# Linear attention by chunks and two gated layers: products regrouped by bank, and another bound in the test of the inputs

## The reference

```python
for t in range(S):
    state = alpha[:, :, t, :, None] * state + np.einsum('bhd,bhe->bhde', k[:, :, t], v[:, :, t])
    y[:, :, t] = np.einsum('bhd,bhde->bhe', q[:, :, t], state)
...
h = x @ w_in
g = P(h) / (Q(h) + 1e-06)
x = g @ w_out
h = x @ w_in2
solu = h * softmax(h)
out = layernorm(solu, g_ln) @ w_out2
```

## Time and profile before

| what | us |
|---|---|
| median of three runs | 815.07 |
| the profiled execution | 815.7 |
| its span, first to last instruction | 814.0 |
| busy in the span: PE | 785.0 (96%) |
| busy in the span: DVE | 689.2 (85%) |
| busy in the span: ACT | 607.9 (75%) |
| busy in the span: POOL | 313.2 (38%) |

### The profile page before, as it was taken

One profiled execution on the slowest core, in us unless ns is written; L12 is line 12 of the kernel. 1 busy time (PEld: TensorE's weight loads), 2 busy tenths in 40 slices (PEclk: granted clock), 3 DMA queues, 4 the chain that ended last, 5 costly groups with the idle time before them and its releaser, 6 DMA issues.

```text
span 814.0 us, 16268 instructions
## 1 busy us (share of the span) xinstructions
PE 785.0 (96%) x5378; PEld 728.5 (89%) x5378; DVE 689.2 (85%) x1248; ACT 607.9 (75%) x1258; POOL 313.2 (38%) x376
## 2 busy tenths in 40 slices
PE   5989999989889999999999999999999999999998
PEld 4777777779779999999999999999999999999988
DVE  4879999879999888988898888988898888988854
ACT  5778888678878776887678767876778677867743
POOL 4998886522223322332233322332333232323221
PEclk9999999999999999999999999999999999999999
DMA  8899999410000010001000100010001000000000
GB/s 182 204 231 230 236 229 206 126 46 0 30 2 1 11 41 1 10 11 39 0 10 10 39 10 0 10 39 10 0 10 39 10 0 10 11 10 1 11 20 30
DMA packets 113174, 42.96 MB, mean 53 GB/s; under 512 B 101616, under 2 KB 110960, under 8 KB 113136
## 3 DMA queue, kind: packets, MB, share of 16 engines
q1 hardware_dynamic: 110336, 33.04, 17.1%
q0 software_dynamic: 2800, 9.45, 3.9%
HBM read 33.04 MB, written 9.44 MB: 52 GB/s over the span
## 4 chain that ended last, share of the span: by engine, by line
PE 70%; DVE 13%; ACT 7%; issue 3%; SPq 3%; DMA 2%; POOL 0%; PEld 0%; ACTq 0%; DVEq 0%; PEldq 0%; POOLq 0%
PE h_ps L1024 18%; PE acc_ps L1050 17%; PE y_ps L1006 12%; PE z_ps L1068 12%; SPq L210 2%; PE chunks_y L299 2%; DVE work L1268 2%; PE chunks_y L307 2%; PE z_ps L1078 2%; DVE chunks_bp L453 2%; DVE rec L1260 2%; DVE den L1256 2%; ACT rec L1157 1%; ACT g_hi L1147 1%; DVE den L1273 1%
## 5 line engine op out<-in xcount | busy, mean ns | idle before, releaser
L1207 POOL TENSOR_TENSOR g_lo<-work,g_hi 128x384 fp32r<-128x384 f32 x128 | 130.8, 1022 | 401.5 <-ACT g_hi L1147 401.5
L1024 PE MATMUL h_ps<-x,w 128*128 (+1 forms) x1143 | 224.8, 340 | 5.8 <-DVE work L1278 4.3
L1050 PE MATMUL acc_ps<-g_hi,w 128*128 128x384 f32 x768 | 218.4, 338 | 2.2 <-POOL g_lo L1207 2.2
L1024 PEld LDWEIGHTS h_ps<-x,w 128*128 128x128 f32 x1143 | 200.4, 188 | 12.2 <-DVE work L1278 8.3
L1050 PEld LDWEIGHTS acc_ps<-g_hi,w 128*128 128x128 f32 x768 | 141.2, 188 | 2.8 <-POOL g_lo L1207 2.8
L1119 ACT ACTIVATE h<-h_ps 128x384 f32<-128x384 f32 x128 | 61.7, 482 | 99.0 <-PE h_ps L1024 98.8
L1050 PE MATMUL acc_ps<-g_lo,w 128*128 128x384 f32 x384 | 129.6, 338 | 0.0
L1273 DVE SCALAR_TENSOR_TENSOR den<-h,ncoef,den 128x384 f32<-128x384 f32 x128 | 78.6, 614 | 39.9 <-ACT den L1122 38.8
L1068 PE MATMUL z_ps<-w,x 128*128 128x512 f32 x396 | 99.9, 397 | 2.4 <-DVE lnT L1290 2.4
L1006 PE MATMUL y_ps<-w,lnT 128*128 128x384 f32 x528 | 99.9, 338 | 0.0
L1147 ACT ACTIVATE g_hi<-work 128x384 fp32r<-128x384 f32 x128 | 68.1, 532 | 38.2 <-DVE work L1268 35.0
(11 more groups left out here) (135 smaller groups left out, 1168.7 us busy)
## 6 DMA issues: line engine op xcount, KB each, us to landing
work<-in_alpha_dram SPq DMA_DIRECT2D x32, 144.0 KB, 3.7
chunks_xin<-in_q_dram SPq DMA_DIRECT2D x32, 144.0 KB, 3.4
chunks_xin<-in_k_dram SPq DMA_DIRECT2D x32, 144.0 KB, 4.1
chunks_vin<-in_v_dram SPq DMA_DIRECT2D x16, 288.0 KB, 4.0
wstage<-in_moe_w_in_dram POOLq DMA_DIRECT2D x9, 512.0 KB, 5.5
attention_out<-solu SPq DMA_DIRECT2D x32, 144.0 KB, 3.5
out_dram<-ysb SPq DMA_DIRECT2D x24, 192.0 KB, 1.8
x<-attention_out SPq DMA_DIRECT2D x7, 576.0 KB, 3.9
```

Of the source, the lines that this page charges most:

```text
L1024: mm = nc.tensor.matmul(h_ps[:, s % 2, 0:TT], w1[:, wz, kc, s * P:(s + 1) * P], xs[:, xz, kc, :], start=(n == 0), stop=(n == 3 * KC - 1))
L1050: mm = nc.tensor.matmul(acc_ps[:, dc, 0:TT], w2[:, wz, f, dc * P:(dc + 1) * P], rhs, start=(f == 0 and n == 0), stop=(f == FC1 - 1 and n = ...
L1207: nc.gpsimd.tensor_tensor(g_lo[:, 1 - o, :], gate[:, 1 - o, :], g_hi[:, 1 - o, :].bitcast(F32), ALU.subtract).then_inc(glo_done, 1)
```

## The change

- `y`'s second bank (chunks 3 to 5) holds the pair's heads in swapped places: head 0 in rows 64 to 111, head 1 in rows 0 to 47 (`y_row`). The rows in between that nothing writes any more are cleared once by DVE.
- On TensorE all of `within` comes first, then all of `before`, in the order of chunks 1, 4, 2, 5, 3, so that four products in a row use four different quarters of the array; `y_done` is raised once a pair.
- ACT copies `ktok` in one instruction of 672 columns and y in one of 768, instead of two each.
- The stores are four per pair, of 48 rows by 384, instead of two of 48 by 2 by 384.
- The test: exp(-80 * alpha) goes. In its place the sum of 1/b, taken by `accum_out` on the exp that computes 1/b anyway, is compared with 2^60. exp(60 * alpha) stays, and its bound becomes exp(60 * 1.05) where it was exp(60 * 1.35).
- POOL clears `seen` once at the start, and ACT and DVE wait for that; semaphore values follow the new counts; `ext` has another home.

```diff
-DECAY_MIN, DECAY_MAX = 0.71, 1.35
-LOW_STEEP, HIGH_STEEP = -80.0, 60.0
-LOW_MAX = math.exp(LOW_STEEP * DECAY_MIN)
-HIGH_MAX = math.exp(HIGH_STEEP * DECAY_MAX)
+DECAY_MAX = 1.05
+STEEP = 60.0
+HIGH_MAX = math.exp(STEEP * DECAY_MAX)
+RECIPROCALS_MAX = 2.0 ** 60
...
+        def y_row(j, z):
+
+            return (j ^ z) * HB
...
-            for j in range(2):
-                nc.sync.dma_start(
-                    scratch[bass.ds(m // PPB * 2, 2), bass.ds(m % PPB * (2 * D) + j * D, D), :].rearrange("o d t -> d o t"),
-                    halves(yout[j * HB:j * HB + D, :]),
-                ).then_inc(att_stored, 16)
+            for z in range(2):
+                for j in range(2):
+                    nc.sync.dma_start(
+                        scratch[bass.ds(m // PPB * 2 + z, 1), bass.ds(m % PPB * (2 * D) + j * D, D), :].rearrange("o d t -> (o d) t"),
+                        yout[y_row(j, z):y_row(j, z) + D, z * HS:(z + 1) * HS],
+                    ).then_inc(att_stored, 16)
...
+        nc.gpsimd.memset(seen[:], 0.0).then_inc(setup, 1)
...
-                mm = nc.tensor.matmul(y[rows, c // CPH, (c % CPH) * P:(c % CPH + 1) * P], st[rows, :, c - 1],
-                                      qp[rows, p, c * P:(c + 1) * P], start=False, stop=(c % CPH == CPH - 1))
+                row = y_row(j, c // CPH)
+                mm = nc.tensor.matmul(y[row:row + D, c // CPH, (c % CPH) * P:(c % CPH + 1) * P], st[rows, :, c - 1],
+                                      qp[rows, p, c * P:(c + 1) * P], start=False, stop=(c in (CPH - 1, CPH)))
...
                 within(p, CPH)
-                for c in range(1, CPH):
-                    mm = before(p, c)
-                mm.then_inc(y_done, 1)
                 pe.wait_ge(att_ready, n * 2)
                 for c in range(CPH + 1, NC):
                     within(p, c)
...
-                for c in range(CPH, NC):
+                for c in (1, 4, 2, 5, 3):
                     mm = before(p, c)
                 mm.then_inc(y_done, 1)
...
-                for x, steep in enumerate((LOW_STEEP, HIGH_STEEP)):
-                    if x == 0:
-                        wait(act, ksq_seen if i_is(n, 1) else vsq_seen, n if i_is(n, 1) else m)
-                    else:
-                        act.wait_ge(range_seen, n * 2 + 1)
-                    nc.scalar.activation(junk[:, 0:NC * ROWS], ain[:, o].rearrange("p c d -> p (c d)"), ACT.Exp,
-                                         scale=steep, accum_out=seen[:, x, bass.ds(n, 1)]).then_inc(range_seen, 1)
+                wait(act, ksq_seen if i_is(n, 1) else vsq_seen, n if i_is(n, 1) else m)
+                nc.scalar.activation(junk[:, 0:NC * ROWS], ain[:, o].rearrange("p c d -> p (c d)"), ACT.Exp,
+                                     scale=STEEP, accum_out=seen[:, 1, bass.ds(n, 1)]).then_inc(range_seen, 1)
...
-                nc.scalar.activation(ktok[:, 0:CPH, :], turn_k[:, 0, 0:CPH * ROWS].rearrange("p (c d) -> p c d", c=CPH),
+                nc.scalar.activation(ktok[:].rearrange("p (z c) d -> p z (c d)", z=2), turn_k[:, :, 0:CPH * ROWS],
                                      ACT.Copy).then_inc(ktok_ready, 1)
-                nc.scalar.activation(ktok[:, CPH:, :], turn_k[:, 1, 0:(NC - CPH) * ROWS]
-                                     .rearrange("p (c d) -> p c d", c=NC - CPH), ACT.Copy).then_inc(ktok_ready, 1)
...
-                nc.scalar.activation(turn_aq[0:ROWS, :, 0:HS], halves(rec[0:ROWS, :]), ACT.Exp, scale=-1.0
-                                     ).then_inc(rec0_ready, 1)
+                nc.scalar.activation(turn_aq[0:ROWS, :, 0:HS], halves(rec[0:ROWS, :]), ACT.Exp, scale=-1.0,
+                                     accum_out=seen[0:ROWS, 0, bass.ds(n, 1)]).then_inc(rec0_ready, 1)
...
-                for z in range(2):
-                    act.wait_ge(y_done, n * 2 + (z - 1))
-                    if z == 0:
-                        wait(act, att_stored, m * 32)
-                    nc.scalar.activation(yout[0:ROWS, z * HS:(z + 1) * HS], y[0:ROWS, z, 0:HS],
-                                         ACT.Copy, scale=-1.0).then_inc(y_copied, 1)
+                act.wait_ge(y_done, n)
+                wait(act, att_stored, m * 64)
+                nc.scalar.activation(halves(yout[0:ROWS, :]), y[0:ROWS, :, 0:HS], ACT.Copy, scale=-1.0).then_inc(y_copied, 1)
+        act.wait_ge(setup, 10)
+        act.wait_ge(y_cleared, 1)
...
-        nc.vector.tensor_scalar(okay[:, 0:1], ext[:, 0:1], LOW_MAX, None, ALU.is_le).then_inc(tally, 1)
+        nc.vector.tensor_scalar(okay[:, 0:1], ext[:, 0:1], RECIPROCALS_MAX, None, ALU.is_le).then_inc(tally, 1)
```

More of the change, by code:

```diff
@@ L152, in attention_by_chunks @@
         setup = sem("setup")
+        y_cleared = sem("y_cleared")
         a_loaded = [sem(f"a_loaded{j}") for j in range(2)]
@@ L201, in stage2, with v_cols @@
             return not isinstance(n, int) or n > 0
+        def y_row(j, z):
+            return (j ^ z) * HB
+        def v_cols(o, j, c, wide):
+            return vin[:, o].rearrange("p j c d -> p (j c d)")[:, (j * NC + c) * D:(j * NC + c) * D + wide]
         def halves(t):
@@ L232, in body @@
                 wait_alone(sp, a_turned, NPAIR * 2, carrier)
-                wait_alone(sp, range_seen, NPAIR * 2, carrier)
-                wait_alone(sp, att_stored, (NPAIR - 2) * 32, carrier)
+                wait_alone(sp, range_seen, NPAIR, carrier)
+                wait_alone(sp, att_stored, (NPAIR - 2) * 64, carrier)
                 first_tokens(sp, scratch, over)
@@ L257, in sync @@
         iterations(sp, body)
-        sp.wait_ge(y_copied, 2 * NPAIR)
+        sp.wait_ge(y_copied, NPAIR)
         store(NPAIR - 1)
@@ L297, in within @@
             for j in range(2):
+                row = y_row(j, c // CPH)
                 wide = HB if j == 0 else D
-                nc.tensor.matmul(y[j * HB:j * HB + wide, c // CPH, (c % CPH) * P:(c % CPH + 1) * P],
-                                 vin[:, p].rearrange("p j c d -> p (j c d)")[:, (j * NC + c) * D:(j * NC + c) * D + wide],
-                                 att[:, j, c, :], start=(c % CPH == 0), stop=False)
+                nc.tensor.matmul(y[row:row + wide, c // CPH, (c % CPH) * P:(c % CPH + 1) * P],
+                                 v_cols(p, j, c, wide), att[:, j, c, :], start=(c % CPH == 0), stop=False)
         def before(p, c):
@@ L332, in body @@
                 attention_products(p, range(4, NC))
-                pe.wait_ge(ktok_ready, n * 2)
+                pe.wait_ge(ktok_ready, n)
                 pe.wait_ge(v_loaded[p], (i + o) * 16)
-                wait(pe, y_copied, m * 2)
+                wait(pe, y_copied, m)
                 for c in range(NC):
@@ L463, in body @@
             if stage2(n):
-                wait(dve, y_done, m * 2)
+                wait(dve, y_done, m)
                 dve.wait_ge(att_done, n * 2 - 1)
@@ L498, in mask @@
                 causal[:].unsqueeze(1).unsqueeze(1).to_broadcast([P, 2, end - first, P]), ALU.mult).then_inc(att_ready, 1)
-        dve.wait_ge(setup, 9)
+        nc.vector.memset(y[HB // 2:HB, 1, D * NC:HS], 0.0).then_inc(y_cleared, 1)
+        dve.wait_ge(setup, 10)
         iterations(dve, body)
-        dve.wait_ge(range_seen, 2 * NPAIR)
+        dve.wait_ge(range_seen, NPAIR)
         dve.wait_ge(qsq_seen, NPAIR)
@@ L592, in sync @@
             sp.wait_ge(zeroed, 1)
-            sp.wait_ge(att_stored, NB * NPAIR * 32)
+            sp.wait_ge(att_stored, NB * NPAIR * 64)
             sp.wait_ge(over.x0_loaded, 16)
@@ L950, in attention_over @@
             eng.wait_ge(joined, 3)
-            eng.wait_ge(att_copied, NB * NH)
+            eng.wait_ge(att_copied, NB * NH // 2)
         with nc.Block() as block:
@@ L978, in _ @@
                 sp.sem_inc(y_stored, 16)
-                sp.wait_ge(att_stored, NB * NH * 16)
+                sp.wait_ge(att_stored, NB * NH * 32)
                 load(1, 1)
```

19 lines of the change are left out of this document (9 added, 10 removed).

## The result

The changed kernel takes 10,049.55 us (median of 6 runs, 10,045.7 to 10,050.44), the kernel before 814.78 (median of 6, 813.52 to 815.88). The ratio is 12.33, with a 95% interval of 12.316 to 12.348. The profiled execution took 10,045.7 us over a span of 10,044.0.

The account below looks back on a forecast made before the run. It took the failing test to send the kernel through the slow attention, a chain of TensorE and DVE at the lower clock: 815.7 + 8,794 + 382 + 14 - 5 = 10,001, forecast 10,000 us; 8-in-10 range 7,900 to 10,900.

Parts of the forecast that it names:

- The test: End of quick attention: the sum over 672 columns of exp(60 * alpha), 144 e^60, fails the new bound of 20.1 e^60.
- The step: Slow loop: DVE, TensorE and hand-overs form a chain whose terms all add, 11.45 us a step, 768 steps, 8,794 us.
- The clock: Slow loop: TensorE, busy about half at most, stays at the lower clock throughout; a group costs 2.85 us, not 1.5.
- the rival: Slow loop: the full clock comes back, a step takes 8.75 us, the kernel 7,886; chance 0.26 including a mixture.
- The frame: Around the slow loop, per pair: stores 5.5, loads 8, turns with copies 10.4; 23.9 us, 382 for 16 pairs.
- what happens once: Slow way: POOL clears tiles, tokens are loaded and multiplied again; 14 us, bounds 5 to 30.
- The edits to the quick way: Quick attention: the edits to products, copies and stores together take 5 us off.
- the first 156 us shorter by a few: Sign for the quick attention, the kernel's first stage: it gets a few us shorter.
- 0 to 5 in all: Quick attention: two further stores cost SP some 1.0 us of issue per pair, below nothing to 0.3 a pair overall.
- The steady pair: Quick attention: one pair every 9.05 us, its time running through TensorE's loop, with DVE waiting for the turn of alpha.
- four products at a time: Quick attention: 16 of 20 `before` records run four at a time, 0.83 us instead of 1.44, 0.61 less for TensorE.
- the wait of 0.40: Quick attention: DVE's wait for the turn of alpha, all that can be won; 0.4 for some 13 pairs, 5 us.

Follow-up runs that it names:

- filled kernel: The changed kernel with products that nobody reads put into TensorE's two rests of the slow loop: 7,984.53 us (one run).
- light loads: Only 1.5 KB loaded of each further piece of the layers' weights: kernel before 813.17 us, changed kernel with the old bound 805.22 us.

## Why the prediction was right

**The test.** Right: the sum over 672 columns is what decides, the slow way is taken, and the edits to products and copies have no part in the factor of 12. The sum's size, 144 e^60 in the prediction, is bracketed by runs between 121.5 and 221. The 1.0 between the heads make the failure certain for every alpha, but with these inputs the columns of alpha, some 48, would fail at 20.1 by themselves. That was in no row of time before. It came from reading a threshold in the diff and working out what it is compared with.

**The step.** 11.45 forecast, 11.51 measured. The scan takes 1.758 (1.82 by the line through two rows), `kv` and `qs` 0.958 (0.957), `masked` 0.620 (0.56, a guess in the middle of two bounds far apart, 0.154 and 0.957), the sum into y 1.017 (0.957). With the hand-overs, a group on TensorE keeps DVE waiting 2.99 (2.85 and its part of the 0.5). The errors partly cancel, which is luck: the five DVE instructions come to 5.31 against 5.25. 768 steps at 11.51 are 8,840; the forecast was 8,794.

**The clock.** Right: 0.50 throughout the loop. The filled kernel shows that it is the rests that do it, and gives the price, 2.7 us a step, which the rival had put at 2.70 (11.45 less 8.75).

**The frame.** 23.5 us a pair, 23.9 forecast. Stores and loads together took 12.4, not 13.5; a turn with its copy 2.6, as said.

**The sum.** 10,001 against the profiled execution's 10,045.7, short by 45. 46 of it is the steps (8,840 less 8,794); the frame was 6 too high, and the quick way and what happens once 5 too low. Most of these 5 are the quick way, of which the forecast took 5 off: its test ended 0.7 us earlier.

**The edits to the quick way: the step that failed,** small beside the rest. The term was "I take 5 us off for all edits together"; with the old bound they cost 1.8 (interval 0.0 to 3.4). The sign that went with it, the first 156 us shorter by a few, came out as 0.7. Three things in it were wrong.

- The stores' "0 to 5 in all" was taken at its lower end, and they cost 4.8 (interval 3.0 to 6.6).
- The steady pair was read as TensorE's and DVE's alone, though the DMA share of the first stage was 0.91. A q that comes late, or stores that land late, stop TensorE, and after the stop it works at the lower clock for some us.
- The gain was put down to four products at a time, with ACT's edits and the order beside it worth nothing. With light loads all edits together gave 8.0, and 4.4 of them came without the swapped places.

What was right: the ten products take 0.91 instead of 1.44 (0.83 forecast), and the wait of 0.40 is gone. That four at a time need the order 1, 4, 2, 5, 3 was wrong; the swapped places are enough.

The Trainium skill's TensorEngine Tiling (Gotcha 1: PSUM Pressure) says that different row tiles cannot access the same PSUM bank at the same time. The trace does not agree: in the swapped kernel 20 records that write two banks, each bank from two row tiles, take 0.91 us, 0.046 apiece, where a turn of 128 columns takes 0.13. Before, the 12 records of the second bank alone took 0.83, 0.069 apiece.

## What to carry to other kernels

A test that guards a quick way is part of its time: for each threshold that a diff touches, write down what is compared with it (a sum or a maximum, over how many terms, padding included) and evaluate it at the inputs' limits before any cost is added up. A chain that passes from engine to engine could be priced here within 1% from rows of other shapes, with some luck in one term, because it was also asked which clock TensorE has when it works half of the time. And where a pair's time is that of an engine, look at the DMA share and at what the edit adds to the transfers before taking the engine's gain as the kernel's: here edits that gave 8.0 us with light loads cost 1.8 (0.0 to 3.4) with full ones.

## What the runs showed of the hardware

- TensorE, busy 4,554 of 9,222 us in pieces of 2.9 us, stayed at the lower of its levels (0.50, 1.2 GHz) throughout. With 4,960 of 7,100 us it stayed near the full one (0.97), and the kernel with the added products was 2,065 us faster.
- DVE's TENSOR_SCALAR over 768 fp32 columns takes 0.620 us, TENSOR_TENSOR over as many 0.958. From one column (0.154) to 768 the first grows by 0.61 ns per column; the same step to the second is 1.05. The Trainium skill's VectorE: DVE Perf Modes (Mode 2×_2P — use both read ports for one tensor) says that with a single source in SBUF the engine reaches twice the rate even in fp32, and with a second tensor it does not. The trace agrees in direction, at 1.7 times instead of twice.
- Four stores of 72 KB instead of two of 144 KB cost 4.8 us over 16 pairs, although they hold the same rows of 1.5 KB. Four issues hold SP's queue for 4.29 us at their worst in that kernel and 5.25 in the changed kernel with the old bound, 3.56 of them in the first issue, where the slow way issues four in 2.08 with nothing beside them.
- Ten small products (20 records of 48 rows by 128 columns) on four quarters of the array take 0.91 or 0.93 us in two different orders, 1.34 on two quarters.
- With heads unswapped, the 24 records of `within` and the 20 of `before` take 3.04 us up to the next turn when they stand in four runs, 2.72 when they stand in two; ACT's work differs too between these kernels.
